# One order for all iterations in a delta-rule recurrence with two expert layers

## The reference

```python
state = zeros(B, H, D, D)                      # B, H, S, D = 4, 8, 768, 48
for t in range(S):                             # k is normalised by its length
    y[:, :, t] = q[:, :, t] @ state
    v_old = k_n[:, :, t] @ state
    state += beta[t] * outer(k_n[:, :, t], v[:, :, t] - v_old)
x = y as [B * S, H * D]                        # 3072 x 384
x = ((x @ w1) * (x @ w2)) @ w3 @ w_out         # inner width 1024
logits = x @ phi                               # 32 slots, 4 for each of 8 experts
d = softmax of logits down the tokens; slots = d.T @ x
slot_out[e] = relu(slots[e] @ e1[e]) @ e2[e]
out = softmax of logits along the slots @ slot_out
```

## Time and profile before

| | |
|---|---|
| runs | 497.6, 498.43, 499.61 us |
| the profiled execution | 500.47 us |
| its span, first to last instruction | 498.7 us |
| TensorE (PE) busy | 451.8 us, 91% |
| VectorE (DVE) busy | 243.0 us, 49% |
| ScalarE (ACT) busy | 227.9 us, 46% |
| GpSimd (POOL) busy | 188.2 us, 38% |
| granted TensorE clock, mean | 0.969 |

### The profile page before, as it was taken

One profiled execution on the slowest core, in us unless ns is written; L12 is line 12 of the kernel. 1 busy time (PEld: TensorE's weight loads), 2 busy tenths in 40 slices (PEclk: granted clock), 3 DMA queues, 4 the chain that ended last, 5 costly groups with the idle time before them and its releaser, 6 DMA issues.

```text
span 498.7 us, 21400 instructions
## 1 busy us (share of the span) xinstructions
PE 451.8 (91%) x9729; PEld 324.1 (65%) x9729; DVE 243.0 (49%) x499; ACT 227.9 (46%) x408; POOL 188.2 (38%) x329
## 2 busy tenths in 40 slices
PE   3675899998999999999999999999999998999982
PEld 3333467776778777778676777677877776754442
DVE  3899686353633637345384245545362422144123
ACT  1323555444455455555454655454654562424112
POOL 1001399811388503887018880168830000000000
PEclk9965999999999999999999999999999999999997
DMA  7999304230006500054000541000080095599949
GB/s 201 383 230 335 92 3 103 88 71 3 4 3 129 129 4 5 2 131 129 4 3 3 106 114 43 4 4 3 4 312 30 3 349 162 205 413 431 422 181 372
DMA packets 21002, 64.96 MB, mean 130 GB/s; under 512 B 2352, under 2 KB 3760, under 8 KB 20016
## 3 DMA queue, kind: packets, MB, share of 16 engines
q1 hardware_dynamic: 20208, 62.71, 38.5%
q10 hardware_dynamic: 704, 0.89, 0.7%
HBM read 58.87 MB, written 4.72 MB: 127 GB/s over the span
## 4 chain that ended last, share of the span: by engine, by line
PE 83%; DMA 8%; issue 3%; DVE 2%; SPq 1%; ACT 1%; DVEq 0%
PE pA L1223 20%; PE pB L1223 20%; PE pKY L1125 5%; DMA arena<-w3t_dram 5%; PE pD L1159 4%; PE pKY L1174 4%; PE pKY L1140 4%; DMA step_slab<-e_dram 3%; PE pT L1241 3%; PE pG L1241 3%; PE pD L1249 2%; PE pT L1109 2%; PE pT L1186 2%; PE pA L1269 1%; PE pG L1109 1%
## 5 line engine op out<-in xcount | busy, mean ns | idle before, releaser
L485 POOL TENSOR_TENSOR prod_p<-prep_slab 128x30 f32<-128x30 f32 (+9 forms) x150 | 76.0, 507 | 45.0 <-DVE prep_slab L820 34.0
L753 DVE TENSOR_TENSOR arena<-a_sb,pB 128x512 f32<-128x512 f32 x41 | 28.1, 686 | 128.2 <-PE pB L1223 125.5
L486 POOL TENSOR_TENSOR prep_slab<-prep_slab,prod_p 128x30 f32<-128x30 f32 (+9 forms) x150 | 81.5, 543 | 11.8
L524 ACT ACTIVATE step_slab<-pKY 32x384 f32<-32x384 f32 x92 | 44.4, 482 | 34.0 <-PE pKY L1174 32.4
L1223 PE MATMUL pB<-whi,xhi 128*128 128x512 f32 x135 | 55.9, 414 | 0.0
L1223 PE MATMUL pB<-whi,xlo 128*128 128x512 f32 x135 | 53.3, 395 | 0.0
L1223 PE MATMUL pB<-wlo,xhi 128*128 128x512 f32 x135 | 53.1, 393 | 0.0
L1223 PE MATMUL pA<-whi,xhi 128*128 128x512 f32 x135 | 51.6, 437 | 0.0
L1223 PE MATMUL pA<-wlo,xhi 128*128 128x512 f32 x135 | 46.8, 399 | 0.0
L1223 PE MATMUL pA<-whi,xlo 128*128 128x512 f32 x135 | 46.4, 398 | 0.0
L466 POOL TENSOR_TENSOR arena<-arena,nrm 128x1152 f32<-128x1152 f32 (+1 forms) x11 | 21.1, 1914 | 49.8 <-DVE prep_slab L842 49.1
(11 more groups left out here) (284 smaller groups left out, 895.2 us busy)
## 6 DMA issues: line engine op xcount, KB each, us to landing
arena<-e_dram SPq DMA_DIRECT2D x7, 1536.0 KB, 14.3
arena<-kq_dram SPq DMA_DIRECT2D x44, 192.0 KB, 5.5
late_w<-e_dram SPq DMA_DIRECT2D x4, 1536.0 KB, 10.8
arena<-kv_dram SPq DMA_DIRECT2D x6, 768.0 KB, 5.4
arena<-kv_dram SPq DMA_DIRECT2D x24, 192.0 KB, 5.9
arena<-w3t_dram SPq DMA_DIRECT2D x2, 2048.0 KB, 20.7
arena<-w_dram SPq DMA_DIRECT2D x1, 4096.0 KB, 14.0
out_dram<-late_w SPq DMA_DIRECT2D x6, 576.0 KB, 5.4
```

What stands on the lines that cost most here:

```text
L485: link(nc.gpsimd.tensor_tensor(pv, a, x, ALU.mult))
L486: link(nc.gpsimd.tensor_tensor(dst, dst, pv, ALU.add))
L524: nc.scalar.activation(xs[quad(b), :], pKY[quad(quarter(g, b) ^ 1), bank(g, b), 0:DM], ACT.Copy).then_inc(y_done, 1)
L753: nc.vector.tensor_tensor(ab_tile(s, p)[:, half * HF:(half + 1) * HF], a_sb[:], up_bank(t, half, 1), ALU.mult).then_inc(ab_done, 1)
```

## The change

The special orders of n = 1 are taken out on all engines, so that steps 4 and 5 are laid as steps 8 and 9 are; `scale(1)` moves from step 4 to step 3 by that. In each iteration's step `s = 0` the first Newton step moves ahead of `ab_mul` of half 1. In the last step (23) `y_step` moves from the middle of the up products of half 1 to the place ahead of `ab_turn` of half 0.

```diff
--- before.py
+++ after.py
@@ -649,9 +649,6 @@
                     z_out(g)
                     if s == 1 and fin:
                         logits_out(n - 1)
-                    if n == 1:
-                        gram_out_at(2)
-                        gram_out_at(3)
                     if g == 1:
                         key_merge(g + 1, 0)
                     if g + 1 < NT:
@@ -659,15 +656,10 @@
                     if s == 1 and fin:
                         act.wait_ge(log_ps, n)
                     abt_out(t, ts, 0)
-                    if n > 1:
-                        gram_out_at(2)
-                        gram_out_at(3)
-                    if n == 1 and s == 0:
-                        a_out(t, 1)
-                        y_out(g)
-                    else:
-                        y_out(g)
-                        a_out(t, 1)
+                    gram_out_at(2)
+                    gram_out_at(3)
+                    y_out(g)
+                    a_out(t, 1)
 
             iterations(body)
             t = NT - 1
@@ -952,18 +944,11 @@
 
                     if t > 0:
                         x_low(t)
-                    if s == 0 and n > 1:
+                    if s == 0:
                         turn_back(n, p)
-                    if s == 1 and fin and prep and n > 1:
+                    if s == 1 and fin and prep:
                         newton(n + 1, 2)
-                    if n == 1 and s == 0:
-                        scale(1)
-                        turn_back(1, p)
-                        mask_at(0)
-                        mask_at(1)
                     r_rows(g, p, s, n)
-                    if n == 1 and s == 1:
-                        set_up_root(2)
                     if s == 1 and fin and prep:
                         set_up_rest(n + 1, q, k)
                     if g == 1:
@@ -975,34 +960,28 @@
                     if s == 2 and fin:
                         row_softmax_a(n - 1)
                         slot_sums(n - 1)
-                    if n != 1:
-                        mask_at(0)
-                        mask_at(1)
+                    mask_at(0)
+                    mask_at(1)
                     ab_mul(t, ts, 0, tp)
-                    if n == 1:
-                        mask_at(2)
-                        mask_at(3)
                     if g == 1:
                         w_low(0, 0)
                     if g == 2:
                         w_low(1, 1)
                     if g < NT - 1:
                         state(g)
-                    if n != 1:
-                        mask_at(2)
+                    mask_at(2)
                     if g == 1:
                         w_low(0, 1)
                     if s == 2 and fin:
                         row_softmax_b(n - 1)
                     if s == 0 and prep:
                         set_up(n + 1, q, k)
-                        if n > 1:
-                            mask_at(3)
-                    if s == 3 and fin and prep:
+                        mask_at(3)
+                        newton(n + 1, 0)
+                    if s == 3 and prep:
                         scale(n + 1)
                     ab_mul(t, ts, 1, tp)
-                    if s == 0 and prep and n > 1:
-                        newton(n + 1, 0)
+                    if s == 0 and prep:
                         newton(n + 1, 1)
                     if g == 2:
                         first_pt(1, 0, STEPS)
@@ -1093,8 +1072,7 @@
                         pe.wait_ge(kq_in[p][r], keys_landed(p, k))
                     if pair > 0:
                         pe.wait_ge(pt_mask, n * STEPS + 2)
-                        if n > 2:
-                            pe.wait_ge(abt_done, t * 2 + 1)
+                        pe.wait_ge(abt_done, t * 2 + 1)
                     else:
                         pe.wait_ge(abt_done, t * 2)
                         pe.wait_ge(xlo_done, t)
@@ -1358,29 +1336,6 @@
                         slot_sum(n - 1, q)
                     if g > 1:
                         ab_turn(t - 1, (s - 2) % STEPS, q if s <= 1 else p, 1, had if s == 0 else made)
-                    if n == 1 and s == 0:
-
-                        up(t, 0, 0, None, 0, 8)
-                        grams(n + 1, q, k1, 0, 0, t)
-                        up(t, 0, 0, None, 8)
-                        up(t, 0, 1, None, 0, 3)
-                        grams(n + 1, q, k1, 0, 1, t)
-                        up(t, 0, 1, None, 3)
-                        solve_rows(g, p, s, n)
-                        up(t, 1, 0, None, 0, 4)
-                        grams(n + 1, q, k1, 1, 0, t)
-                        up(t, 1, 0, None, 4, 8)
-                        grams(n + 1, q, k1, 1, 1, t)
-                        up(t, 1, 0, None, 8)
-                        state_step(g, p, k, s, n)
-                        ab_turn(t, ts, tp, 0, made - 1)
-                        up(t, 1, 1, None, 0, 2)
-                        y_step(g, p, s)
-                        up(t, 1, 1, None, 2)
-                        pe.wait_ge(s_done, g + 3)
-                        logits(n - 1, 0, FC // 2)
-                        x_turn(g)
-                        continue
                     if s == 0 and prep:
 
                         up(t, 0, 0, None, 0, 5)
@@ -1402,6 +1357,8 @@
                         up(t, 0, 1, sums, ahead)
                     if g < NT - 1:
                         state_step(g, p, k, s, n)
+                    else:
+                        y_step(g, p, s)
                     ab_turn(t, ts, tp, 0, had + 2 if s == 0 and prep else had)
                     if s == 0 and prep:
                         up(t, 1, 0, None, 0, 4)
@@ -1414,7 +1371,8 @@
                         up(t, 1, 1, None, 3)
                     else:
                         up(t, 1, 0, None, 0, 6)
-                        y_step(g, p, s)
+                        if g < NT - 1:
+                            y_step(g, p, s)
                         up(t, 1, 0, None, 6)
                         up(t, 1, 1)
                     if s == 0 and fin:
```

## The result

Thirteen runs of the changed kernel have a median of 495.98 us (494.35 to 498.14), thirteen of the kernel before one of 499.61 us (497.17 to 501.87). The ratio is 0.9931, 95% interval 0.991 to 0.9953: 3.5 us faster. Ratios leave out executions more than 1.5% longer than the fastest of their kernel (five of twelve in e7, one in e11, two of the kernel before beside e5 to e8), medians do not. The forecast was 493.6 us, 4.8 less than the median then shown, a ratio of 0.9903: just outside the first interval, inside the second. The time of 495.98 lies just above the range, which ended at 495.9. So the sign is right, and the size is too large by more than a third, 4.8 against 3.5 us.

The account below looks back on a forecast made before the run. TensorE's work, 83% of the chain, was taken as the bound. Gains 1.53 + 0.89 + 1.38 + 1.0 = 4.8 us off the 498.43 us median gave 493.6 us, range 490.7 to 495.9.

Parts of the forecast that it names:

- What bounds the kernel, clock, tail: TensorE is 83% of the chain, clock 1.00 is no term, and all time gained at TensorE reaches the end.
- Step 4, term 1.53 us: Common order makes step 4 look like step 16: 22.13 - 20.60 = 1.53 us gained; ends 0.97 and 3.13.
- the wait for line 740: In step 4 TensorE waits 0.97 us for VectorE's rows; written some 4 us earlier, this stall goes.
- the borders: New instruction blocks due about every 126 records; step 4's stalls of 1.01 and 0.62 us should become like step 16's.
- 0.97 us if both stalls stay: Lower end of step 4's gain, if both its instruction-fetch stalls remain.
- Scaling in step 3, 0: scale(1) ahead of tile 2's last product, behind GpSimd's solve: cost 0, some 0.5 us to spare.
- The third rival: Slower: in step 3 scale(1) waits for the solve, delaying product and turn; 501.1 us at 8 us late; chance 0.04.
- Newton, 0.89 + 1.38 us: Shorter stalls ahead of state products: 0.89 us in step 5, 3 x 0.46 = 1.38 in steps 9, 13, 17.
- rival 1: No fetch stall in step 4 and Newton's first step wholly hidden: 7.5 us gained, 490.9 us; chance 0.2.
- Last step, 1.0 us: Step 23's output products moved into TensorE's idle slot save 1.0 us; ends 0.7 and 1.02.
- rival 2: Newton move does nothing, step 4 keeps both stalls: 2.1 us, 496.3; only one of these: about 3.2, 495.2; chance 0.2.

Follow-up runs that it names:

- e7: The kernel of e4 with ten fewer filler products at the very start (FILLERS 37 for 47); 500.4 us, ratio 0.9985.
- e11: The kernel of e4 run again unedited; 495.14 us, ratio 0.9927.
- e5: The kernel of e4 with ten more filler products at the very start (FILLERS 57 for 47); 496.57 us, ratio 0.9963.
- e8: The kernel of e4 with scale(1) put back into step 4, ahead of the turn of the solved system; 493.99 us, ratio 0.9901.
- e12: The changed kernel with GpSimd's solve of iteration 1 lengthened by three operations that write scratch; 496.57 us in one run.
- e1: The kernel before with only the order of iteration 1 changed, Newton step and output products at their old places; 497.49 us, ratio 0.9984.
- e9: The changed kernel run again unedited; 494.42 us, ratio 0.992.
- e4: The changed kernel with GpSimd's select made to wait for the first Newton step as well; 493.63 us, ratio 0.9897.
- e6: The kernel of e4 with thirty more filler products at the very start (FILLERS 77 for 47); 498.5 us, ratio 0.9997.

## Why the prediction was too large

- **What bounds the kernel, clock, tail.** Right: the granted clock is 1.00 in the steps as before (0.50 and 0.60 were seen behind the stalls of over 3 us in e12 and e7), and what is gained at TensorE arrives at the end.
- **Step 4, term 1.53 us.** This is the step that failed: "So step 4 should look like step 16, not like step 8: 22.13 - 20.60 = 1.53 us gained." The half on the wait for line 740 held, 0.97 us. The half on the borders did not. Their places were forecast right, at 340 and 465 records; their lengths were taken from one execution of each of two steps as if they belonged to the place, and the one at 340 was put at next to nothing, like the 0.20 us at record 344 of step 16, since it comes "after the up products' relief". That relief was too short: TensorE ran the stride ahead of it in 3.1 us, and stood 0.78 us for the packet. The same border costs 0 to 0.85 us in the executions of the new order, the one at 465 0.69 to 1.24 us where it is not 0 (e12). The new order paid 0.97 to 2.02 us at borders, not 0.6 us less than the 0.74 to 1.63 of the old one. Step 4 was 21.78 us on average before (22.13, 21.85, 21.85, 21.29) and 21.28 in changed, e1 and e9: 0.5 us gained (0.6 with e4, e8 and e11). Even the lower end, "0.97 us if both stalls stay", was none, since a stall that stays can grow.
- **Scaling in step 3, 0.** Off by little. The spare of 0.5 us was read from an execution whose step 3 held a border stall of 0.73 us; where that is shorter or the solve ends later, TensorE arrives sooner and waits: the turn is 0.2 us late in the changed kernel, 0.4 in e11, and 0.7, 0.6 and 1.8 in e5, e6 and e7. The third rival happens in small, then. Its price of one for one is right for the turn; in e12 the clock added 1 us to it.
- **Newton, 0.89 + 1.38 us.** Right. Step 5 gained 0.83, steps 9, 13 and 17 together 1.58 in the first pair of profiles. The working by way of the select held in detail: multiply 0.71 us, done 0.03 us behind the select; e4 shows the cause, since with the select moved away the multiply takes 0.19 us. This held back 1.0 us, the gain of e4's steps. It is not what kept rival 1 away: that needed 3.13 us from step 4, and e4 ran at 493.63 us, not at 490.9.
- **Last step, 1.0 us.** Right: 0.94 us at the end over nine executions.
- **Rivals.** What came is the half of rival 2 in which both stalls of step 4 stay and the Newton move works. The prediction priced one half of it at "about 3.2 us"; by its own terms this half is 0.97 + 0.89 + 1.38 + 1.0 = 4.2 us, so that price was near the measured 3.5 by luck.
- **Borders elsewhere.** Step 12's 0.54 us more in the first profile is chance: 19.50 to 20.33 in seven executions of the new order, 19.74 to 20.00 in four of the old one.

With 0.5 in the place of 1.53 the sum is 3.8 us; measured were 3.5 and 4.0. The forecast in microseconds was also anchored to a median of three runs, 498.43, where thirteen gave 499.61. From there the same sum gives 494.8 us, so the step from the ratio to the time made the miss look larger in microseconds (2.4 us) than the gains were off (1.3 us).

## What to carry to other kernels

A stall inside a block whose members wait for nothing can belong to the count of instructions and not to the code at that place, as all of them did here: note its record number, compare it with the next one, look for the packet of the instruction queue that ends just before it, and treat its length as a draw for each execution, with a price between zero and the longest seen. When a small operation is moved into a gap of one queue, look which engine works in that gap; VectorE had the time, but its multiply ended only with GpSimd's select. And where one queue gets a wait for a slow engine ahead of urgent work, measure the spare in several executions, for a stall elsewhere may be what makes it. A wait of over 3 us at TensorE cost more than itself here, since the granted clock was down for 3 to 4 us behind it.

## What the runs showed that I had not expected

The longest border stall lies ahead of the loop. In the timeline of TensorE before:

```profile
46.44 0.33 PE L1109 MATMUL pB<-arena 48*32 48x64 f32 x3 [6.09 <-issue]
```

and in e6, with 60 records more ahead of it:

```profile
45.26 0.26 PE L1087 MATMUL pB<-arena 48*32 48x64 f32 x1 [5.42 <-issue]
```

The windows up to there, before and e6:

```profile
0.00:46.40 46.40, 24.55 (x604) 14.90 (x605) 33.61 (x97) 9.70 (x18) 1.58 (x11) 0.80 0.98 278
```

```profile
0.00:45.20 45.20, 26.66 (x732) 17.00 (x733) 30.05 (x86) 9.62 (x18) 1.58 (x11) 0.83 0.98 280
```

Record 604 is 8 strides ahead of 1610, and 732 one stride behind 604; the DMA engines are 98% busy over that stretch. A border thus costs 0 to 1.3 us in quiet steps, 1.49, 1.59 and 3.35 us in e7 beside loads of weights, and 5.0 to 6.5 us beside several at the start. What is late there is the start of the packet and not the packet: before, TensorE stops at 40.35 us, the packet starts at 43.82 and takes 1.20 us, and TensorE goes on at 46.44. That the load of instructions queues behind the weights is my reading of this; no run here moved the loads, so it wasn't shown, nor whether those 6 us can be had back.

Step 17 keeps 0.25 us that steps 5, 9 and 13 lose in e4. VectorE idles 0.25 us ahead of line 812 there, and waits for nothing visible. All ten executions with the common order have this gap, and none of the four with the old order of iteration 1 (0.03 to 0.04 us), so it came with the order: step 17 lasts 16.01 us in e1 against 15.80 before. Its cause is open.
